# A tuned Fourier mixing and feed-forward kernel: its 47-point transforms in quarters of the array

## What is computed

```python
def _attn_ref(x, w_r, w_i, b_r, b_i):          # x: 2 x 3008 x 256, float32
    X = np.fft.rfft(x, axis=1)
    Xr, Xi = (X.real.astype(np.float32), X.imag.astype(np.float32))
    Yr = Xr @ w_r - Xi @ w_i + b_r
    Yi = Xr @ w_i + Xi @ w_r + b_i
    lam = 0.01
    Yr = np.sign(Yr) * np.maximum(np.abs(Yr) - lam, 0.0)
    Yi = np.sign(Yi) * np.maximum(np.abs(Yi) - lam, 0.0)
    return np.fft.irfft(Yr + 1j * Yi, n=x.shape[1], axis=1)
...
# then two layers on the 6016 x 256 result: h = x @ w_in, an activation, @ w_out
```

## Time and profile before

| | us |
|---|---|
| median of 3 runs | 1176.28 |
| lowest and highest run | 1175.95, 1177.82 |
| the profiled execution | 1175.93 |
| its span, first to last instruction | 1173.8 |

### The profile page before, as it was taken

The page is one execution under the profiler, slowest core; times in us unless marked ns, Lnnn a source line. Parts: engine busy times, 40 slices in busy tenths (PEclk is TensorE's granted clock), DMA queues, the critical chain, the costliest instruction groups (busy, mean ns, idle before and its releaser), DMA issues.

```text
span 1173.8 us, 20998 instructions
## 1 busy us (share of the span) xinstructions
PE 1167.1 (99%) x6946; PEld 1138.4 (97%) x6946; DVE 887.2 (76%) x1678; ACT 852.6 (73%) x1880; POOL 687.0 (59%) x718
## 2 busy tenths in 40 slices
PE   9999999999999999999999999999999999999998
PEld 3899999999999999999999999999999999999998
DVE  4787777777777777777777787778778787878776
ACT  3445567777676777777677688888888787878776
POOL 1017647577565767666556566665757575756554
PEclk9999999999999999999999999999999999999999
DMA  9788411111121201202005500000000000000000
GB/s 354 228 258 267 153 55 44 52 42 54 54 70 40 68 28 41 95 27 68 19 5 177 197 19 2 27 1 28 1 28 1 27 1 27 1 27 1 14 15 27
DMA packets 41644, 77.61 MB, mean 66 GB/s; under 512 B 4672, under 2 KB 21184, under 8 KB 41536
## 3 DMA queue, kind: packets, MB, share of 16 engines
q1 hardware_dynamic: 38784, 67.82, 17.5%
q10 hardware_dynamic: 2752, 8.45, 2.0%
HBM read 45.97 MB, written 30.28 MB: 65 GB/s over the span
## 4 chain that ended last, share of the span: by engine, by line
PE 99%; DVE 0%; DMA 0%; issue 0%; SPq 0%; ACT 0%
PE bank L1272 45%; PE bank L1180 39%; PE bank L1146 6%; PE bank L1165 2%; PE bank L1120 2%; PE bank L1156 2%; PE bank L1131 2%; DMA x_sb<-x 0%; DVE g_sb L985 0%; DVE y_sum L881 0%; DVE bank L970 0%; DVE y_tile L1007 0%; ACT xc_hi L653 0%; DVE r L905 0%; DVE bank L975 0%
## 5 line engine op out<-in xcount | busy, mean ns | idle before, releaser
L519 POOL TENSOR_TENSOR g_lo<-g_sb,g_hi 128x376 fp32r<-128x376 f32 x510 | 505.4, 1002 | 362.5 <-ACT g_hi L784 361.6
L1272 PE MATMUL bank<-g_hi,w_out_hi 128*128 128x376 f32 x1024 | 342.8, 335 | 0.0
L1272 PE MATMUL bank<-g_hi,w_out_lo 128*128 128x376 f32 x1024 | 341.5, 333 | 0.0
L1180 PE MATMUL bank<-xc_hi,w_in_hi 128*128 128x376 f32 x896 | 302.5, 338 | 0.1
L1180 PE MATMUL bank<-xc_hi,w_in_lo 128*128 128x376 f32 x896 | 299.6, 334 | 0.0
L1180 PE MATMUL bank<-xc_lo,w_in_hi 128*128 128x376 f32 x896 | 299.0, 334 | 0.0
L784 ACT ACTIVATE g_hi<-g_sb 128x376 fp32r<-128x376 f32 x512 | 261.1, 510 | 45.6 <-DVE g_sb L985 28.7
L1272 PE MATMUL bank<-g_lo,w_out_hi 128*128 128x376 f32 x1024 | 259.6, 334 | 0.0
L1272 PEld LDWEIGHTS bank<-g_hi,w_out_hi 128*128 128x128 f32 x1024 | 192.2, 188 | 0.5
L1272 PEld LDWEIGHTS bank<-g_hi,w_out_lo 128*128 128x128 f32 x1024 | 192.7, 188 | 0.0
L1272 PEld LDWEIGHTS bank<-g_lo,w_out_hi 128*128 128x128 f32 x1024 | 184.2, 188 | 0.0
(11 more groups left out here) (84 smaller groups left out, 1528.8 us busy)
## 6 DMA issues: line engine op xcount, KB each, us to landing
gc<-group_consts SPq DMA_DIRECT2D x24, 256.0 KB, 4.5
zt<-slots_scratch SPq DMA_DIRECT2D x24, 256.0 KB, 4.0
inverse_scratch<-v_sb SPq DMA_DIRECT2D x24, 256.0 KB, 3.3
ut<-inverse_scratch SPq DMA_DIRECT2D x16, 384.0 KB, 5.1
slots_scratch<-a_sb ACTq DMA_DIRECT2D x15, 384.0 KB, 5.6
out<-y_tile SPq DMA_DIRECT2D x30, 188.0 KB, 1.9
x_sb<-x SPq DMA_DIRECT2D x17, 256.0 KB, 6.8
prep_raw<-wpack SPq DMA_DIRECT2D x16, 256.0 KB, 2.9
```

What stands on the lines that cost most here:

```text
L519: pool.tensor_tensor(g_lo[kind][:, :], g_sb[n % 3][:, :], g_hi[kind][:, :].bitcast(f32), ALU.subtract)\
L1180: done = pe.matmul(bank_of[:, 0:N], w_part[:, fp, w * P:(w + 1) * P], x_part[q % 2][:, xs, :], start=first and n == 0, stop=last_one and n ...
L1272: last = pe.matmul(acc_bank[k][c][:, 0:N], w[:, fp, upper * D + c * P:upper * D + (c + 1) * P], g_part[kind][:, :], start=first and n == 0 ...
```

## The change

A tile of x is now 47 rows for each of the two halves, which lie in partitions 0 to 46 and 64 to 110. `fwd_sb` is 128 by 64: the same 47 by 48 matrix for each half, at partition 0 and at 64. `real47` makes four products of 512 columns for a tile, one for each half of the rows (h) and each half of the columns (c); each uses 47 rows and 64 columns of the array, and writes 64 partitions (from 64 c) of the bank of h. So a bank holds one half of the rows, with both halves of the columns one above the other. The copies take 112 partitions for 96.

All 16 tiles have a place of their own in SBUF; there are no fills and no waits for places. x lies in DRAM by pairs of tiles, `(8, 2, 47, 2, 1024)`. `LOADS` lists nine loads for each half h: tile 0, tile 1, then seven pairs; SyncE issues those of h = 0, ScalarE those of h = 1 (four at once, one more behind each odd tile). A row of a pair is 8 KB, in one piece in DRAM and in SBUF. Nothing is padded: each load has 47 rows.

A store takes two tiles of one half c, 48 partitions with two pieces of 4 KB each, two such stores for a pair of tiles, all of them by ScalarE. The order of the 64 positions in `slots_scratch` changes by that, and the rows of the group matrices are permuted on the host to match (`place`). Tile 15 is transformed with the others, ahead of `forward(0)`. SyncE's program is its nine loads with fwd behind the first, the matrices of pair 0, the wait for batch 0, and the rest as before.

```diff
 DC = D // P
-FIRST_TILES = TILES - 1
-LATE_TILES = {1: FIRST_TILES}
-LATE_STORES = {2 * n + 2: TILES_PER_BATCH + n for n in range(TILES_PER_BATCH)}
-FULL_TILES = 1
-X_SLOTS = 8
-VECTOR_FILLS, POOL_FILLS = (2, 4, 7), (1, 3, 5, 6)
-
-
-
-PARTS = ((0, P // 2, slice(0, P, 2)), (P // 2, ROWS_PAD, slice(1, P, 4)))
-
-LEAD = 6
-SCALAR_LOADS = tuple(range(FULL_TILES, X_SLOTS)) + tuple(range(TILES_PER_BATCH + 4, TILES))
+
+
+QUARTER = P // 2
+SLOTS_47 = N1 + 1
+A_ROWS = QUARTER + SLOTS_47
+
+LOADS = ((0, 1), (1, 1)) + tuple((t, 2) for t in range(2, TILES, 2))
+EARLY_LOADS = 4
+LATE_STORES = {2 * n + 2: (TILES_PER_BATCH + n // 2 * 2, n % 2) for n in range(TILES_PER_BATCH)}
...
         for half in range(HALVES):
-            fwd[half:ROWS:2, 2 * slot + half] = f
+            fwd[QUARTER * half:QUARTER * half + N1, slot] = f
...
+
+    place = np.arange(N2).reshape(HALVES, TILES_PER_BATCH, 2, 2).transpose(1, 2, 0, 3).reshape(N2)
+    fwd_g = fwd_g.reshape(GROUPS, 2, N2, P)[:, :, place].reshape(GROUPS, P, P)
...
-    az_rows = az.rearrange("b (p j) d -> b p (j d)", j=J)
     vz_rows = vz.rearrange("b (p j) d -> b p (j d)", j=J)
+    az_slots = az.rearrange("b (s q m) d -> b s q (m d)", s=SLOTS_47, q=2 * TILES_PER_BATCH)
...
-        x_sb = sb("x_sb", [P, X_SLOTS, TILE_COLS], scope=step_a)
-        a_sb = sb("a_sb", [ROWS_PAD, TILES, TILE_COLS], scope=step_a)
+        x_sb = sb("x_sb", [P, TILES, TILE_COLS], scope=step_a)
+        a_sb = sb("a_sb", [P, TILES, TILE_COLS], scope=step_a)
...
         wm_lo_ready = sem("wm_lo_ready")
-        x_in = [sem(f"x_in{i}") for i in range(TILES)]
-        x_half_in = sem("x_half_in")
+        x_in = [sem(f"x_in{i}") for i in range(len(LOADS))]
...
-        def load_rows(eng, t, part):
-
-            if t in VECTOR_FILLS:
-                eng.wait_ge(zeros_by_vector, VECTOR_FILLS.index(t) + 1)
-            elif t in POOL_FILLS:
-                eng.wait_ge(zeros_by_pool, POOL_FILLS.index(t) + 1)
-            else:
-                eng.wait_ge(a_done, 2 * (t - X_SLOTS) + 2)
-            lo, hi, partitions = PARTS[part]
-            eng.dma_start(x_sb[partitions, t % X_SLOTS, :], x[x_row(t) + lo:x_row(t) + hi, :]).then_inc(x_in[t], 16)
+        def load_x(eng, n, h):
+
+            first, count = LOADS[n]
+            rows = slice(QUARTER * h, QUARTER * h + N1)
+            eng.dma_start(x_sb[rows, first:first + count, :], x[first // 2, h, :, first % 2:first % 2 + count, :])\
+               .then_inc(x_in[n], 16)
+
+        def store_a(eng, t, c):
+
+            b, q = t // TILES_PER_BATCH, 2 * (t % TILES_PER_BATCH) + c
+            eng.wait_ge(a_left, t + 2)
+            eng.wait_ge(a_right, t + 2)
+            eng.dma_start(az_slots[b, :, q:q + 3:2, :], a_sb[QUARTER * c:QUARTER * c + SLOTS_47, t:t + 2, :])\
+               .then_inc(a_stored[b], 16)
...
-            sp.dma_start(x_tile(0)[:, 0:HALF_COLS], x[0:P, 0:HALF_COLS]).then_inc(x_half_in, 16)
+            load_x(sp, 0, 0)
             sp.dma_start(fwd_sb[:, :], fwd47).then_inc(fwd_in, 16)
-            sp.dma_start(x_tile(0)[:, HALF_COLS:], x[0:P, HALF_COLS:]).then_inc(x_in[0], 16)
-            for t in range(FULL_TILES, TILES - 2):
-                load_x(t)
+            for n in range(1, len(LOADS)):
+                load_x(sp, n, 0)
             load_matrices(0)
-            load_x(TILES - 2)
-            t = TILES_PER_BATCH - 1
-            sp.wait_ge(a_right, t + 1)
-            sp.dma_start(az_rows[0, 0:ROWS_PAD, t * TILE_COLS + HALF_COLS:(t + 1) * TILE_COLS],
-                         a_tile(t)[:, HALF_COLS:]).then_inc(a_stored[0], 16)
-            load_x(TILES - 1)
-            sp.wait_ge(a_stored[0], 16 * (TILES_PER_BATCH + 1))
+            sp.wait_ge(a_stored[0], 16 * TILES_PER_BATCH)
...
-            for t in POOL_FILLS:
-                pool.memset(x_tile(t), 0.0).then_inc(zeros_by_pool, 1)
...
             def copy_a(t, bank_a):
                 act.wait_ge(a_done, 2 * t + 1)
-                act.activation(a_tile(t)[:, 0:HALF_COLS], bank_a[0:ROWS_PAD, :], ACT.Copy).then_inc(a_left, 1)
-
-            def store_a(t):
-                b, q = t // TILES_PER_BATCH, t % TILES_PER_BATCH
-                act.wait_ge(a_left, t + 1)
-                if t == TILES_PER_BATCH - 1:
-                    act.dma_start(az_rows[b, 0:ROWS_PAD, q * TILE_COLS:q * TILE_COLS + HALF_COLS],
-                                  a_tile(t)[:, 0:HALF_COLS]).then_inc(a_stored[b], 16)
-                    return
-                act.wait_ge(a_right, t + 1)
-                act.dma_start(az_rows[b, 0:ROWS_PAD, q * TILE_COLS:(q + 1) * TILE_COLS],
-                              a_tile(t)).then_inc(a_stored[b], 16)
-
+                act.activation(a_tile(t)[0:A_ROWS, 0:HALF_COLS], bank_a[0:A_ROWS, :], ACT.Copy).then_inc(a_left, 1)
+
+            load_x(act, 0, 1)
 
             act.wait_ge(half_ready, 1)
             act.activation(neg_alpha[:, 0:1], half[:, :], ACT.Copy)
-            for t in range(FULL_TILES, X_SLOTS):
-                load_rows(act, t, 1)
-            for t in range(FIRST_TILES):
+            for n in range(1, EARLY_LOADS):
+                load_x(act, n, 1)
+            for t in range(TILES):
                 copy_a(t, a_bank[(2 * t) % 4])
-                if t < TILES_PER_BATCH:
-                    store_a(t)
-                if t >= LEAD and t + LEAD in SCALAR_LOADS:
-                    load_rows(act, t + LEAD, 1)
-                if t == TILES_PER_BATCH:
+                if t % 2:
+                    if t < TILES_PER_BATCH:
+                        store_a(act, t - 1, 0)
+                        store_a(act, t - 1, 1)
+                    n = EARLY_LOADS + t // 2
+                    if n < len(LOADS):
+                        load_x(act, n, 1)
+                if t == TILES_PER_BATCH + 1:
                     act.dma_start(wm_raw[:, :], wmix).then_inc(wm_in, 16)
...
-                if s in LATE_TILES:
-                    copy_a(LATE_TILES[s], a_bank[0])
...
                 if s in LATE_STORES:
-                    store_a(LATE_STORES[s])
+                    store_a(act, *LATE_STORES[s])
...
-            for t in VECTOR_FILLS:
-                dve.memset(x_tile(t), 0.0).then_inc(zeros_by_vector, 1)
 
             def copy_a(t, bank_a):
                 dve.wait_ge(a_done, 2 * t + 2)
-                dve.tensor_copy(a_tile(t)[:, HALF_COLS:], bank_a[0:ROWS_PAD, :]).then_inc(a_right, 1)
-
-            for t in range(FIRST_TILES):
+                dve.tensor_copy(a_tile(t)[0:A_ROWS, HALF_COLS:], bank_a[0:A_ROWS, :]).then_inc(a_right, 1)
+
+            for t in range(TILES):
                 copy_a(t, a_bank[(2 * t + 1) % 4])
...
-                if s in LATE_TILES:
-                    copy_a(LATE_TILES[s], a_bank[1])
...
-            def real47(t, banks):
-                for part, copied in enumerate((a_left, a_right)):
-                    if t == 0 and part == 0:
-                        pe.wait_ge(x_half_in, 16)
-                    else:
-                        pe.wait_ge(x_in[t], 16 if t < FULL_TILES else 32)
+            def real47(t):
+                pe.wait_ge(x_in[load_of(t)], 32)
+                for h, copied in enumerate((a_left, a_right)):
                     if t >= 2:
-                        pe.wait_ge(copied, t - 1 if t < FIRST_TILES else t)
-                    pe.matmul(banks[part][0:ROWS_PAD, :], fwd_sb[:, :], x_tile(t)[:, part * HALF_COLS:(part + 1) * HALF_COLS],
-                              start=True, stop=True).then_inc(a_done, 1)
+                        pe.wait_ge(copied, t - 1)
+                    rows = slice(QUARTER * h, QUARTER * h + N1)
+                    for c in range(2):
+                        last = pe.matmul(a_bank[(2 * t + h) % 4][QUARTER * c:QUARTER * (c + 1), :], fwd_sb[rows, :],
+                                         x_sb[rows, t, c * HALF_COLS:(c + 1) * HALF_COLS], start=True, stop=True)
+                    last.then_inc(a_done, 1)
...
-            for t in range(FIRST_TILES):
-                real47(t, [a_bank[(2 * t + part) % 4] for part in range(2)])
+            for t in range(TILES):
+                real47(t)
             for s in range(STEPS):
                 forward(s)
-                if s in LATE_TILES:
-                    real47(LATE_TILES[s], a_bank[0:2])
...
-    order = list(range(0, P, 2)) + list(range(1, P, 4))
-    used = sorted(order)
-    tiles = np.zeros((TILES, P, TILE_COLS), x.dtype)
-    tiles[:, used[:ROWS]] = x.reshape(BATCH, ROWS, TILES_PER_BATCH, TILE_COLS).transpose(0, 2, 1, 3)\
-                             .reshape(TILES, ROWS, TILE_COLS)
-    rows = [tiles[:FULL_TILES].reshape(-1, TILE_COLS), tiles[FULL_TILES:, order].reshape(-1, TILE_COLS)]
+    tiles = x.reshape(BATCH, N1, HALVES, TILES_PER_BATCH // 2, 2, TILE_COLS).transpose(0, 3, 2, 1, 4, 5)
```

More of the change, by code:

```diff
@@ L76, in transform_constants @@
     n1 = np.arange(N1)
-    fwd = np.zeros((ROWS_PAD, ROWS_PAD))
+    fwd = np.zeros((P, QUARTER))
     inv = np.zeros((ROWS_PAD, ROWS))
```

(28 more changed lines are left out.)

## The result

The changed kernel takes 1396.07 us (median of 4 runs, 1394.27 to 1396.31) against 1176.40 for the kernel before on the same chip (4 runs): a ratio of 1.186, 95% interval 1.184 to 1.188. The forecast was 1401.0, range 1275 to 1440. The profiled execution took 1396.18 us with a span of 1394.4.

What follows compares the result with a forecast made beforehand. TensorE bounds the kernel, with DMA nearly even in the first stage. First forward product 257 instead of 31.6 (+225.4), next steps +2, late tile -1.7: 1175.93 + 225.7 = 1401.6 us, range 1275 to 1440.

Steps and rivals of the forecast that it cites:

- Which term decides: Loads of x before the first forward product: 47-row transfers all pass over one DMA engine, +225.4 us; chance 0.80.
- Rival D: Loads of x: 47 rows on one engine, but each queue or transfer on another; 1282 us, down to about 1210; chance 0.04.
- The size of the term: First stage: 6.50 MB on one engine at 26.0 GB/s takes 250 us, 253 with start and landing.
- The last pair: End of the first stage: both tiles come at 253 us, take 4 us at 1.2 GHz; first forward product 257.
- The late tile: Tile 15 moves ahead of the first forward step, so 1.7 us leave the chain behind it.
- Quarters: Products of the 47-point transforms: four quarters run together, 0.86 us a tile, the sixteen 13.7 instead of 27.5.
- Rival C: First stage: loads spread over engines but quarters don't overlap, 3.44 us a tile, 55 for sixteen; 1203.6 us; chance 0.05.
- Cover of queues: ScalarE's copies, stores and load per pair of tiles take 2.4 us, covered by 3.7 us of transfers.
- the values for batch 0: Sign in the first stage: their load comes near half of 257 us, no longer on the chain.
- Rival B: First stage: loads spread over all engines at 416 GB/s, first forward product 29.7; 1172.3 us (1169 to 1175); chance 0.11.

Runs made afterwards that it cites:

- half and half: Changed kernel with 48-row loads for h = 1 (ScalarE) only, h = 0 keeping 47 rows: 1293.99 us in one run.
- kernel with filler: Kernel with the old loads plus an unused whole-array product of zeros behind each of tiles 1 to 14: 1186.45 us, ratio 1.0074.
- kernel with the old loads: Changed kernel with loads, places and fills of the kernel before; quarters of 64 rows, paired stores and tile 15's move stay: 1184.00 us, ratio 1.0059.
- 128-row kernel: Changed kernel with both halves in one load of 128 rows (64 + 64 with padding), nine loads by SyncE: 1183.32 us, ratio 1.005.

## Why the prediction was right, and where its steps were off

*Which term decides.* Right, and shown: 47 rows, 1396; 48 rows, 1200; 45 and 2 rows, 1198; half and half, 1294. The reasoning from equal shares in the earlier trace rows had no row of its own kind and 0.80 was given to it. By what the Trainium skill says in DMA: Bandwidth & Descriptors, section Why a DMA increments its semaphore by 16 and not by 1 (the largest divisor up to 16; lowest-numbered engines), 47 gives one engine, 48 sixteen, 45 fifteen and 2 two, and two issuing queues share the one. The runs with 47, with 48 and with 47 in one half agree. With 45 and 2 rows the share is 0.96 in the mean from 5 to 25 us, for 1.02 with 48: more than one engine for certain, and what fifteen of sixteen would give. Rival D, an engine for each queue, falls with them, at 26 GB/s for both queues together.

*The size of the term.* 250 us for 6.50 MB at 26.0 GB/s. The last pair landed at 246.4 and the flow began near 2: about 244 us, or 26.6 GB/s, 2% better and within what I had left open.

*The last pair.* 4 us at half clock were given; 3.69 were measured (records of 1057 ns, where the earlier trace rows have 592 for products at full clock). First forward product: forecast 257, measured 250.1, the sum of both deviations and the landing. These 6.9 us too many are partly offset by 1.8 too few behind it (late tile, below).

*The late tile.* The step that failed, in small. I took 1.7 us off, since tile 15 leaves the next stage. In before that tile was no bare cost: it filled the wait for the split of the mixing weights. From the end of the early tiles to `mix(0)` before needs 2.61 us with the late tile in it (31.77 to 34.38), the change 3.1 (250.16 to 253.28), in which TensorE has only `forward(0)` and `forward(1)`, while ScalarE copies tile 15, makes `wm_hi`, and VectorE `wm_lo` and `xt_lo`: the chain above. The same 3.1 stand in the kernel with filler at full clock (40.81 to 43.93). So the move brought a loss of 0.5, not a gain of 1.7. (A `forward` is two products, four records, and not four products as the section on the kernel before has it: the eight records in the earlier trace rows are the first two.) With the half clock at `mix(0)` (2.90 for 1.67 us, then 1.69) the rest behind the first forward product is 1394.4 - 250.1 = 1144.3 against 1173.8 - 31.6 = 1142.2: +2.1 where I had +0.3.

*Quarters.* They overlap. At full clock and with 64 rows a tile takes 1.02 us between work of the whole array, less than the 1.72 of two at a time. With 47 rows a tile takes 1.98 us alone and 1.77 in a row. By itself that would fit two at a time at full clock as well; it is the half clock (last section) that makes it four at a time. But "0.86 a tile, the sixteen 13.7" holds in no run, since with 47 rows none of the records ran at full clock: 1057 ns in the median of each kernel with 47-row products, also where they followed each other without a gap. The halving in time was given back by the halved clock. Rival C's 3.44 is met nowhere.

*Cover of queues.* "ScalarE's queue per pair 2.4 us, covered" was wrong as a price, though it cost nothing in this kernel: issue durations of before don't hold when the engine behind them is backed up. The timeline of the changed kernel (SyncE and ScalarE):

```profile
11.45 37.67 SPq L318 DMA_DIRECT2D x_sb<-x  x2
...
18.32 1.98 PE L1088 MATMUL bank<-x_sb,fwd_sb 47*64 47x512 f32 x8 [14.80 <-DMA fwd_sb<-fwd]
...
128.77 29.05 ACTq L326 DMA_DIRECT2D slots_scratch<-a_sb  x2
158.99 28.05 SPq L334 DMA_DIRECT2D gc<-group_consts  x1
200.62 0.40 SPq L340 DMA_DIRECT2D zt<-slots_scratch  x1
```

One load of matrices takes 28 us to issue. I had expected the values for batch 0 near half of the 257 us; they are issued at 200.6, still ahead of need. In the kernel with the old loads the same effect does reach TensorE.

*Rival B.* Its condition, spread loads, was met in six kernels with the change's own loads or close to them, and its 1172 in none. The rate was wrong: 416 GB/s, measured 178 to 237 at first in the five of them whose loads don't reach over all partitions, and even with the old loads 318 from 20 to 25 us where the earlier trace rows have 413. With 48 written for 47, rival B would have been my forecast, a gain, and wrong by 28 us.

*What stays open.* With the old loads the rest of the change costs 7.2 us (6.3 between the profiled spans, 1180.1 and 1173.8). `mix(0)` starts 4.4 us later, of which 0.5 is the late tile, and takes 1.2 longer at half clock. Some 4 us lie in a stage that moves 312 to 338 GB/s at a share near 1. The stores of 48 rows in one half of the partitions are the obvious suspect, but the 128-row kernel has the same stores and keeps 418 to 428 from 15 to 30 us. What differs there is the pieces of 8 KB, the single queue of loads, and places for all tiles. No run tells these apart.

## What to carry to other kernels

Before any other number, factor the row count of each transfer: the price of 47 rows was 220 us, that of 48 or of 45 and 2 some 20, so cut an odd count into parts or pad it. Then look at which partitions the rows lie in, with GB/s beside the busy share, for the share reads 1.0 in either case. And where TensorE and transfers limit a stage alike, as here, a faster TensorE gained nothing: it waited, and its clock halved. Work that fills a wait at the seam of two stages, like the late tile here, is free where it stands; look what it hides before it is moved.

## What the runs showed of the hardware that I had not expected

A small transfer is held by the one engine as well: `fwd_sb` (one row above, idle 14.80) was issued at 1.14, took 17.1 us to land (2.4 in the earlier trace rows) and let the first product start only at 18.32. Its part on the shared engine stood behind 47-row loads, as I read it: with 48-row loads it lands in 4.3 us. An issuing instruction lasts longer when the DMA engines behind it are backed up: 24.3 us in the median for SyncE's loads of x in the changed kernel, up to 2.4 us for stores in the kernel with the old loads, against 0.31; other work of that engine waits, a copy included. A change between whole array and quarters seems to cost something: 1.02 + 1.05 for a tile and a filler, where whole-array products follow each other at 0.86 and quarters in a row at 1.77 for a doubled 0.88.

The records of the 47-row products last 1057 ns while the granted clock reads 1.00 in the same stretches, even in the 128-row kernel, where TensorE has no gap for 24 us; with 64 rows the fastest last 588 ns, and where those slow down (2.05 us a tile) the column does read 0.50. I take the 47-row records for half clock, 1.2 GHz, against the column. The forward products right behind the last tile, which use the whole array, take twice the 1.05 us of the earlier trace rows:

```profile
250.06 2.07 PE L1100 MATMUL bank<-gc,zt 128*128 128x128 f32 x8
```

In the 128-row kernel the products of `mix` start 0.21 us apart at 39 to 45 us and 0.12 apart from there on, while the column reads 1.00 in both. And in before it reads 1.00 from 0 to 5 us, where records take 1057 to 1168 ns. So in these traces a 1.00 ahead of the column's first fall doesn't tell the clock; the durations do. Why the clock doesn't rise under products of 47 rows stays open.
